# Attention and two MLPs on one core: other token pieces, and the first piece's turns in other banks

## The reference

```
scores = (1/8) * q @ k.T                              # 576 x 576 for each of 32 heads
kth    = the 32nd largest score of each row
attn   = exp(where(scores >= kth, scores, -1e9) - rowmax); attn /= sum + 1e-9
x      = (attn @ v), heads side by side               # 2304 x 512
x      = (sigmoid(x @ w_gate) * (x @ w_val)) @ w_out  # first MLP
h      = relu(x @ w_in);  out = (h * h) @ w_out2      # second MLP
```

## Time and profile before

| | |
|---|---|
| median of 3 runs | 1231.99 us |
| profiled execution | 1234.21 us |
| its span | 1232.4 us |
| PE busy | 1164.7 us, 95% |
| DVE, ACT, POOL busy | 848.1, 740.2, 627.4 us |
| first MLP matmul | 95.91 us after the start |

### The profile page before, as it was taken

How to read it: one execution, slowest core, us unless ns; L and a number is a source line. 1 busy time by engine, 2 the same in 40 slices (tenths; PEclk the granted TensorE clock), 3 DMA queues, 4 the chain that set the end, 5 groups by cost and what they waited for, 6 DMA issues and landing times.

```text
span 1232.4 us, 21820 instructions
## 1 busy us (share of the span) xinstructions
PE 1164.7 (95%) x7520; PEld 988.5 (80%) x7520; DVE 848.1 (69%) x1756; ACT 740.2 (60%) x1758; POOL 627.4 (51%) x539
## 2 busy tenths in 40 slices
PE   3459998999999999999999999999999999999999
PEld 1347887889988988888888777777777888888999
DVE  7988997978779967878997677788854544610121
ACT  5877777876778766656775665577554443621231
POOL 4865667766667745445663454356533342530220
PEclk9769999999999999999999999999999999999999
DMA  9874767677666685565556555545555455556997
GB/s 333 317 281 142 253 208 247 220 258 263 212 231 225 231 293 197 166 193 192 167 197 208 209 171 180 184 155 189 171 176 189 166 181 181 178 180 229 364 362 266
DMA packets 89245, 270.13 MB, mean 219 GB/s; under 512 B 9904, under 2 KB 15024, under 8 KB 89136
## 3 DMA queue, kind: packets, MB, share of 16 engines
q1 hardware_dynamic: 89136, 268.74, 63.8%
HBM read 228.33 MB, written 40.37 MB: 218 GB/s over the span
## 4 chain that ended last, share of the span: by engine, by line
PE 80%; ACT 8%; POOL 6%; DVE 3%; issue 2%; DMA 1%; SPq 0%; ACTq 0%; DVEq 0%; POOLq 0%
PE ps L553 21%; PE ps L555 20%; PE ps L554 20%; PE ps L494 7%; PE ps L458 5%; PE ps L474 5%; POOL below L784 3%; PE ps L539 3%; ACT scores L585 2%; DVE work L721 2%; DVE top L719 1%; ACT probs L604 1%; POOL stage L779 1%; ACT below L590 1%; ACT below L597 1%
## 5 line engine op out<-in xcount | busy, mean ns | idle before, releaser
L784 POOL TENSOR_TENSOR below<-scores,below 128x576 f32<-128x576 f32 x144 | 205.4, 1426 | 294.7 <-ACT below L597 291.6
L719 DVE MAX8 top<-work 128x8 f32<-128x576 f32 x432 | 313.0, 752 | 5.0
L553 PE MATMUL ps<-xy_hi,ring 128*128 128x512 f32 (+3 forms) x800 | 291.1, 364 | 0.0
L555 PE MATMUL ps<-xy_hi,ring 128*128 128x512 f32 (+3 forms) x800 | 282.8, 354 | 0.0
L554 PE MATMUL ps<-xy_lo,ring 128*128 128x512 f32 (+3 forms) x800 | 282.5, 353 | 0.0
L721 DVE MATCH_REPLACE8 work<-top,work 128x576 f32<-128x576 f32 x288 | 213.8, 743 | 0.0
L553 PE MATMUL ps<-g_hi,ring 128*128 128x512 f32 (+3 forms) x560 | 203.0, 362 | 0.0
L555 PE MATMUL ps<-g_hi,ring 128*128 128x512 f32 (+3 forms) x560 | 197.8, 353 | 0.0
L554 PE MATMUL ps<-g_lo,ring 128*128 128x512 f32 (+3 forms) x560 | 197.6, 353 | 0.0
L553 PEld LDWEIGHTS ps<-xy_hi,ring 128*128 128x128 f32 x800 | 150.8, 189 | 24.2 <-issue 9.4
L555 PEld LDWEIGHTS ps<-xy_hi,ring 128*128 128x128 f32 x800 | 150.8, 189 | 15.9
(11 more groups left out here) (58 smaller groups left out, 1734.5 us busy)
## 6 DMA issues: line engine op xcount, KB each, us to landing
ring<-w_split SPq DMA_DIRECT2D x318, 512.0 KB, 3.7
wring<-w_in SPq DMA_DIRECT2D x113, 256.0 KB, 4.0
w_split<-stage SPq DMA_DIRECT2D x46, 512.0 KB, 4.3
w_split<-ring SPq DMA_DIRECT2D x22, 512.0 KB, 2.9
vt<-v_in SPq DMA_DIRECT2D x16, 480.0 KB, 5.5
heads_in<-qk_in SPq DMA_DIRECT2D x16, 336.0 KB, 4.4
vt<-v_in SPq DMA_DIRECT2D x16, 320.0 KB, 3.9
heads_in<-qk_in SPq DMA_DIRECT2D x16, 240.0 KB, 4.0
```

Of the source, the lines that this page charges most:

```text
L553: nc.tensor.matmul(dst, w_hi, hi[:, k, 0:WIDTH[c]], start=first, stop=False)
L555: mm = nc.tensor.matmul(dst, w_lo, hi[:, k, 0:WIDTH[c]], start=False, stop=final)
L719: nc.vector.max(out=best, in_=sc if step == 0 else wk).then_inc(sel_step[t % 2], 1)
L784: nc.gpsimd.tensor_tensor(out=below[:, t % 2, :], in0=scores[:, t % PLACES, :], in1=below[:, t % 2, :], op=ALU.subtract).then_inc(mask_don ...
```

## The change

1. The pieces have 192, 320, 384, 512, 512 and 384 tokens instead of 192, 384, 448, 512, 512 and 256. A piece is now a list of ranges of batches: piece 1 comes from batch 1, and piece 2 is the rest of batch 0. Pieces 3 and 4 lie over two batches, and their outputs are stored in two transfers. There are still 64 full and 16 half units, 144 tiles, 150 slots and 816 matmuls a piece. The MLPs start in slots 15, 37, 61, 93, 125 and 149.
2. For units of piece 0 the turn goes to the accumulators' banks 5 to 7. Normalise, turn and product are each a slot earlier (tile + 2, + 2, + 3), and such a turn waits for no copy of scores. Its product now waits for the `copy_x` of the unit before.
3. Ahead of the first MLP the weight splits are spread over slots 0 to 13. ACT begins a slot with the comparison and copies scores behind it; `copy_pt` moves behind the exponential (except in slot 14). POOL splits a slot after ACT, between `mask` and `normalise`. DVE inverts behind a later pass. SP's loads and stores for the splits are also a slot later against ACT's splits.

```diff
-CHUNK_BLOCKS = (3, 6, 7, 8, 8, 4)
+PIECES = (((0, 0, 3),), ((1, 0, 5),), ((0, 3, 6),), ((1, 5, 4), (2, 0, 4)), ((2, 4, 5), (3, 0, 3)), ((3, 3, 6),))
...
-MASK, NORM, TURN, PROD = 2, 3, 3, 4
-MLP_AT = [CHUNK_END[c] + (5 if c < NW else 6) for c in range(NC)]
+MASK = 2
+MLP_AT = [CHUNK_END[c] + (4 if c == 0 else 6) for c in range(NC)]
+NORM_AT, TURN_AT, PROD_AT = {}, {}, {}
+for _t in range(NT):
+    _late = UNITS[TILES[_t][0]][0] > 0
+    NORM_AT[_t + 2 + _late] = _t
+    if _t in UNIT_AT:
+        TURN_AT[_t + 2 + _late] = PROD_AT[_t + 3 + _late] = UNIT_AT[_t]
...
-    SPLIT_AT.setdefault(min(2, MLP_AT[0] - (NPRE + 1) // 2) + _k // 2, []).append(_k)
+    SPLIT_AT.setdefault(_k * (MLP_AT[0] - 1) // NPRE, []).append(_k)
...
+        def early(u):
+            return UNITS[u][0] == 0
+
+        def turned(u, k, n):
+
+            bank = (5 if early(u) else 2) + k // 4
+            return ps[:, bank, P * (k % 4):P * (k % 4 + n)]
...
-                        sp.dma_start(out[m, :, START[c]:START[c] + WIDTH[c]],
-                                     act_buf[:, m % 2, 0:WIDTH[c]]).then_inc(out_stored[m % 2], 16)
+                        col = 0
+                        for b, at, blocks_n in PIECES[c]:
+                            token, cols = b * SEQ + B64 * at, B64 * blocks_n
+                            sp.dma_start(out[m, :, token:token + cols],
+                                         act_buf[:, m % 2, col:col + cols]).then_inc(out_stored[m % 2], 16)
+                            col += cols
...
-                wait(pe, s_copied, max([t + 1 for t in range(NT) if TILES[t][1] == 1
-                                        and FIRST_OF[TILES[t][0]] - SCORE <= END[u] + TURN], default=0))
-
-                wait(pe, x_done, u)
+                if not early(u):
+
+                    wait(pe, s_copied, max([t + 1 for t in range(NT) if TILES[t][1] == 1
+                                            and FIRST_OF[TILES[t][0]] - SCORE <= TURN_SLOT[u]], default=0))
+
+                    wait(pe, x_done, u)
...
                 pe.wait_ge(pt_copied, u + 1)
+                if early(u):
+
+                    wait(pe, x_done, u)
...
+            for s in range(min(SCORE_AT) + 1, MLP_AT[0]):
+
+                if 0 <= s - MASK:
+                    find_below(s - MASK)
+                    enlarge(s - MASK)
                 if s - 1 in SCORE_AT:
                     for t in tiles_of(SCORE_AT[s - 1]):
                         copy_scores(t)
+                if s in PROD_AT and s == MLP_AT[0] - 1:
+                    copy_pt(PROD_AT[s])
+                if 0 <= s - MASK:
+                    exp(s - MASK)
+                if s in PROD_AT and s < MLP_AT[0] - 1:
+                    copy_pt(PROD_AT[s])
+                for k in SPLIT_AT.get(s, []):
+                    split_weights(k)
+                if s in PROD_AT:
+                    copy_x(PROD_AT[s])
...
```

More of the change, by code:

```diff
@@ L23 @@
 KFULL = NBLK // 2
-CHUNK_BLOCKS = (3, 6, 7, 8, 8, 4)
-NC = len(CHUNK_BLOCKS)
+PIECES = (((0, 0, 3),), ((1, 0, 5),), ((0, 3, 6),), ((1, 5, 4), (2, 0, 4)), ((2, 4, 5), (3, 0, 3)), ((3, 3, 6),))
+NC = len(PIECES)
 NW = 1
-WIDTH = [B64 * n for n in CHUNK_BLOCKS]
-START = [sum(WIDTH[:c]) for c in range(NC)]
+WIDTH = [sum(B64 * n for b, at, n in pieces) for pieces in PIECES]
 NMAX = max(WIDTH)
@@ L36 @@
 for _c in range(NC):
[L37 to L41, removed]
+    _col = 0
+    for _b, _at, _n in PIECES[_c]:
+        GROUPS += [(_c, _b, _p, _at, _n, _col) for _p in range(PAIRS)]
+        _col += B64 * _n
 NG = len(GROUPS)
@@ L210 @@
     for _p in range(PAIRS):
[L211 removed]
+        _s = max(PROD_SLOT[X_UNIT[_c][_p]] + 1, slot_of_block(_c - 1, OUT0 - 1) + 1)
         X_AT.setdefault(_s, []).append((_c, _p))
[L213 removed]
+V_AT = {FIRST_TILE[_g - 1] + 4: _g for _g in range(2, NG)}
 SPLIT_AT = {}
 for _k in range(NPRE):
[L217 removed]
+    SPLIT_AT.setdefault(_k * (MLP_AT[0] - 1) // NPRE, []).append(_k)
 def attention_mlps(nc, qk, v, w, w_split, out):
@@ L351, in wait_stored, with stores_ahead @@
                 eng.wait_ge(ring_stored[ring_place(k)], 16 * ring_stores(k))
+        def stores_ahead(c, m):
+            ahead = sum(len(PIECES[i]) for i in range(min(c, NC))) * (NM // 2)
+            return 16 * (ahead + (len(PIECES[c]) * (m // 2) if c < NC else 0))
         block = ctx.enter_context(nc.Block())
@@ L425, in _ @@
                     load_v(V_AT[s])
+                for k in SPLIT_AT.get(s - 2, []):
+                    load_weights(k + WPLACES)
                 for k in SPLIT_AT.get(s - 1, []):
-                    load_weights(k + WPLACES)
-                for k in SPLIT_AT.get(s, []):
                     store_parts(k)
@@ L433, in _ @@
             for i in range(2):
[L434 removed]
+                sp.wait_ge(out_stored[i], stores_ahead(NC, NM + i))
         @block.tensor
@@ L443, in score @@
                 wait(pe, s_copied, FIRST_OF[u])
-                if part == 1:
-                    wait(pe, pt_copied, sum(END[v] + TURN < FIRST_OF[u] - SCORE for v in range(NU)))
+                ahead = sum(TURN_SLOT[v] < FIRST_OF[u] - SCORE for v in range(NU))
+                if part == 1 and ahead and not early(ahead - 1):
+                    pe.wait_ge(pt_copied, ahead)
                 q = B64 * GROUPS[g][4]
@@ L472, in turn @@
                 for k in range(KFULL + 1 if half else NBLK):
-                    dst = ps[:, T0 + k // 4, P * (k % 4):P * (k % 4) + P] if k < 8 else ps[:, LAST, 0:P]
-                    mm = nc.tensor.transpose(dst, both[:, P * k:P * k + P], ident[:, :])
+                    mm = nc.tensor.transpose(turned(u, k, 1), both[:, P * k:P * k + P], ident[:, :])
                 mm.then_inc(transposed, 1)
@@ L682, in _ @@
                         copy_scores(t)
-                if s < 0:
-                    continue
-                if 0 <= s - MASK < NT:
+                if s in PROD_AT and s == MLP_AT[0] - 1:
[6 more added lines that the diff above has]
+                    split_weights(k)
+                if s in PROD_AT:
+                    copy_x(PROD_AT[s])
+            for s in range(MLP_AT[0], SLOTS):
+                if s - 1 in SCORE_AT:
+                    for t in tiles_of(SCORE_AT[s - 1]):
+                        copy_scores(t)
+                if s - MASK < NT:
                     find_below(s - MASK)
                     enlarge(s - MASK)
-                for c, n in blocks_of(SHARES[s - 1][2]) if s else []:
+                for c, n in blocks_of(SHARES[s - 1][2]):
                     evac(c, n)
-                if s - PROD in UNIT_AT:
-                    copy_pt(UNIT_AT[s - PROD])
+                if s in PROD_AT:
+                    copy_pt(PROD_AT[s])
                 for c, p in X_AT.get(s, []):
                     split_x(c, p)
-                if 0 <= s - MASK < NT:
+                if s - MASK < NT:
                     exp(s - MASK)
-                for k in SPLIT_AT.get(s, []):
-                    split_weights(k)
                 for c, n in blocks_of(SHARES[s][0]):
                     evac(c, n)
-                if s - PROD in UNIT_AT:
-                    copy_x(UNIT_AT[s - PROD])
+                if s in PROD_AT:
+                    copy_x(PROD_AT[s])
                 for c, n in blocks_of(SHARES[s][1]):
@@ L761, in _ @@
             for s in range(SLOTS):
[L762 to L765, removed]
+                select_both(s, [0, 1])
+                if s in NORM_AT and s >= MLP_AT[0]:
+                    invert(NORM_AT[s])
                 for c, n in blocks_of(SHARES[s - 1][2]) if s else []:
@@ L768, in _ @@
                 select_both(s, [2])
+                if s in NORM_AT and s < MLP_AT[0]:
+                    invert(NORM_AT[s])
                 for c, n in blocks_of(SHARES[s][0] + SHARES[s][1]):
@@ L834, in _ @@
                     mask(s - MASK)
-                if 0 <= s - NORM < NT:
-                    normalise(s - NORM)
+                for k in SPLIT_AT.get(s - 1, []):
+                    split_weights(k)
+                if s in NORM_AT:
+                    normalise(NORM_AT[s])
                 for c, n in blocks_of(SHARES[s - 1][2]) if s else []:
```

28 lines of the change are left out of this document (13 added, 15 removed).

## The result

The changed kernel takes 1244.5 us (median of 6 runs, 1240.2 to 1247.2); the kernel before takes 1232.9 us beside it (1232.0 to 1233.9). The ratio is 1.009, with a 95% interval of 1.007 to 1.011. It is slower, by 0.9%; I had forecast 1224.8, in a range from 1216 to 1236. The profiled execution took 1240.2 us, the lowest of the six, and has a span of 1238.4 us, 6.0 more than the kernel before. The medians differ by 11.6 us, so the trace holds about half of the loss; the rest differs from run to run.

What follows compares the result with a forecast made beforehand. The prediction saw a 95.9 us start set by ACT's list, then PE working through a fixed amount with small holes. Start -6.0, matmuls -1.1, attention +0.7, holes -1.1 and end +0.3 gave -7.2: 1224.8 us from 1232.0, range 1216 to 1236.

Steps and rivals of the forecast that it cites:

- The holes of piece 1: Beside piece 1's MLPs: PE work per slot 6.98 us against 6.94 before, so holes of 5.0 us (-0.9).
- my full-clock sum: PE's work in piece 1: MLPs 122.4 us plus attention 45.1 us over 24 slots, 6.98 us each.
- nothing: At the stores: eight more output stores through SP, which mostly waits for others, cost no time.
- The start, -6.0: Ahead of the first MLP: its first matmul comes at 89.9 us, 6.0 us earlier than before.
- the start does not move: Rival, ahead of the first MLP: ACT waits half a microsecond a slot for stage places; 1230.8 us, chance 0.12.
- the first period: First three slots after slot 2, ahead of the first MLP: 17.6 us, with nothing added for the lower clock.
- given back by exposed copies of turned units: Ahead of the first MLP: hidden score copies' gain is lost to turned-unit copies; the dropped slot wins less than 5.9 us.
- the straight line: Rival, MLP matmuls of 320 columns: 146.7 ns each, not 150.0, gaining 2.7 us more; 1222.1 us, chance 0.12.
- The holes of pieces 0, 2 and 3: Beside these MLPs: piece 0 holes 5.0 us (-6.5), piece 2 6.5 us (+6.3), piece 3 unchanged.
- The slower rival: Pieces 1 and 2: attention uncovered, 0.46 us lost a slot, holes 25.8 us not 11.5; 1239.1 us, chance 0.15.
- The sum: Whole kernel: start -6.0, MLP matmuls -1.1, attention +0.7, holes -1.1, end +0.3, together -7.2 us.
- The signs that I had named: Forecast is wrong if the start is later than 93 us or pieces 1 and 2 together exceed 392 us.

Runs made afterwards that it cites:

- e3: The changed kernel with pieces 1 and 2 exchanged (384 tokens of batch 0 before 320 of batch 1): 1250.5 us, ratio 1.0138 to the kernel before.
- e4: The changed kernel with SP issuing piece 1's stores of split weights two blocks later: 1234.0 us, ratio 1.0002 to the kernel before.
- e6: e4 with ACT copying the turned unit before the exponential in all slots ahead of the first MLP: 1225.4 us, ratio 0.9934 to the kernel before.

## Why the prediction was wrong, point by point

- **The holes of piece 1: the step that failed.** I took "the same rate, 5.0" because PE has as much work in a slot as before. Measured: 188.8 us against 119.7 + 45.1 = 164.8 of PE's work, 24.0 of holes: 16.6 with PE idle, and 7.4 by which PE was busy for longer than my full-clock sum. Half of the 13.7 us at the lower clock is 6.9, so nearly all of the 7.4 is clock, a cost that my sum had only ahead of the first MLP. The rate that counts here is not PE's work in a slot but the time in a block, since loads, splits and stores go block by block: 2.86 us of PE a block before, 2.64 in e3 and 164.8 / 68 = 2.42 in the changed kernel go with 5.9, 12.5 and 24.0 us of holes. My sum did not have SP's queue in it beyond the output stores ("nothing"); e4 shows 10.1 us of these holes in this piece's stage (10.6 of the kernel's time), lower clock included, to come from a load behind a waiting store. What makes the other 13.9 is not settled; rows of PE waiting for ACT's copies of turned units (9.7 us in the changed kernel, 6.8 in e4) are the largest group left.
- **The start, -6.0: failed, 0.0 measured.** My adding had the right rate at the lower clock: 19.3 us in three slots, and in the trace ACT's comparisons stand at 54.63 and 73.89, 19.26 apart. Two terms were off. I left out the wait for a stage place, which I had as a condition of the rival "the start does not move"; it was one wait of 4.6 us and not half a microsecond a slot. It makes slot 2 take 9.25 us (comparisons at 13.17 and 22.42), not 4.5. And I let the first period run at full clock; it took 19.3 us too (comparisons at 22.42 and 41.67), 1.7 more. I had read the 0.75 of the earlier trace rows as the clock in the whole stretch. The changed kernel's trace has 1.00 for 20 to 43 us, and yet eight score matmuls last 2.29 us there, where the earlier trace rows has 1.61:

```profile
24.58 2.29 PE L484 MATMUL ps<-heads_in 64*128 64x288 f32 x8 [10.96 <-ACT scores L614]
```

  So early in these traces the clock column can't be trusted, and the length of a matmul has to be read. e6 shows the step that I named ("given back by exposed copies of turned units") to be worth 8 us of the start.
- **320 columns: the straight line was right.** The rows have eight spacings in 1.18 us, 147 ns each:

```profile
319.69 0.31 PE L582 MATMUL ps<-g_hi,ring 128*128 128x320 f32 x1
...
320.87 0.31 PE L584 MATMUL ps<-g_hi,ring 128*128 128x320 f32 x1
```

  So the rule of the Trainium skill that I weighed (page "TensorE: Matmul & The Clock Gate", section "Back-to-back issue gap") has the slope right at 320 columns, and 448 stays the exception. The same section of the Trainium skill gives this rule for a single matmul's gap, and for a stream of weight loads and matmuls about 131 ns at 512 columns; here such a stream has 226.7 ns at 512, so the measurement decides. With 146.7 ns for 320 columns my sum gives 3.8 us won by the matmuls, not 1.1.
- **The holes of pieces 0, 2 and 3: right in sign, better than forecast.** Piece 0 took 134.2 us (2.7 of holes; I had 5.0), piece 2 203.8 (1.4; I had 6.5), piece 3 247.6 (250.0 before; I had no change). The slower rival, uncovered attention in pieces 1 and 2, did not happen in piece 2. In piece 1 the 10.1 us of SP's queue are another mechanism; the 13.9 us that are left, 0.58 a slot, are more than the 0.46 that the rival asks, and no run tells whether they are the rival's. Its 1239.1 us stands close to the profiled 1240.2 by luck, since the rival put 14.7 of its 25.8 us of holes into piece 2. In e3's piece 2 the holes are 0.27 us a slot at 5.6 us of PE a slot, which fits that rival; no run isolates it.
- **The sum.** -7.2, corrected by +6.0 (start), +19.0 (piece 1), -2.7 (320 columns), -2.3, -5.1 and -2.4 (pieces 0, 2 and 3), is +5.3; the spans differ by +6.0. So two terms made the miss, piece 1 by far the larger, and errors of 12.5 us the other way hid a part of it. That the median is 4.4 us over the profiled execution is in no trace; it stays open. The slowest of the six runs had the lowest clock of them (0.971, the profiled one 0.983).
- **The signs that I had named.** Both came: the start is later than 93 us, and pieces 1 and 2 together take 392.6 us, over 392.

## What to carry to other kernels

When a piece of work is made narrower or faster, list every chain that advances with it, the queue that issues its loads too, and compare the time per step, not only the bound engine's work. In a list of transfers that is issued in order, a load that is needed soon should not stand behind a store that waits for another engine. And a slot saved in a list is worth what the engine that sets the slot's length gives: look for what became exposed when an instruction moved out of a wait. And look at the clock of each stage beside its idle time: in piece 1 the lower clock cost PE 7.4 us on top of 16.6 idle.

## What was not expected of the hardware

Matmuls of 448 columns are spaced by 206.7 ns in most runs of them, 6.7 more than the line through 256, 320, 384 and 512 columns (120.0, 146.7, 173.3, 226.7 ns); 320, as odd a multiple of 64, is on the line. It isn't so everywhere: behind the next turn four spacings of 448 columns take 0.81 us, 202.5 ns each, and what makes the difference no run shows.

```profile
502.33 0.36 PE L554 MATMUL ps<-xy_lo,ring 128*128 128x448 f32 x1
...
503.14 0.36 PE L555 MATMUL ps<-xy_hi,ring 128*128 128x448 f32 x1
```
